# Two-scale attention and two feed-forward layers: four pairs of the first batch in flight instead of two

## The chip, the cores and the metric

The kernel runs on one core of one Trainium2 chip. The metric is the time of one execution on the device in microseconds; the time before is 996.45 us, the median of 3 runs (994.6 to 997.91).

## What is computed

The inputs are q, k and v of 4 batches, 8 heads, 576 tokens and head size 64, and two pairs of weights. Everything is fp32.

```
def sm_attn(qq, kk, vv):  softmax(scale * qq @ kk.T) @ vv, with 1e-9 added to the row sum
q_d, k_d, v_d = means of each 4 tokens of q, k, v          # 144 coarse tokens
out_up    = repeat(sm_attn(q_d, k_d, v_d), 4)              # the coarse scale
out_local = sm_attn(q, k, v) masked to |i - j| < 4         # the local scale
x = (out_up + out_local), heads side by side               # 2304 x 512
x = leaky(x @ w_in1) @ w_out1      # leaky(h) = max(0.01 h, h); w_in 512 x 2048, w_out 2048 x 512
y = x @ w_in2;  out = (y - tanh(y)) @ w_out2
```

## The kernel before

Attention works on pairs of heads: a pair of one batch fills 128 partitions (2 x 64), and there are 16 pairs, four to a batch. The work of a pair is written as 17 steps, 0 to 16, and every engine has its own part of a step (`attention(step, s, i)` in each engine's block; s is the set of buffers, i the count of its use). TensorE turns q and k token groups (steps 0 to 3, line 364), makes the local scores (4, line 371) and the coarse ones (6, line 438), turns the scaled probabilities (11 to 14, lines 390 and 395) and multiplies them with v (15 and 16, lines 403 and 411). ScalarE copies from PSUM and takes the exponentials. VectorE sums q and k over four tokens (3 and 4, lines 815 and 823), adds the mask `band`, takes maxima and sums, subtracts (6, line 833), inverts (8 and 9), and combines both scales into `xT` (15 and 16, line 803). GpSimd sums v over four tokens (step 5, line 985, three instructions), and scales the local (9, line 992) and the coarse probabilities (10, line 997).

The first batch is done before any feed-forward work. `batch0()` writes out its order: at each slot every pair in flight does one step; pair set A starts at slot 0, set B at slot BEHIND = 5, each set handles two pairs one after the other, so there are 39 slots. Within a slot the young steps (below 6) go first. In its last slots set A does the first four steps (HEAD) of the fifth pair. B's buffers lie in `xT` beyond the first batch's columns.

Layer 1 is computed in 8 tiles of 288 tokens. A tile goes through 16 chunks f of the hidden dimension: `hidden1(tile, f)` makes the hidden chunk in `ph1`, `down1(tile, f)` adds its product with w_out into `acc` two chunks later. fp32 is kept by splitting each operand in a high part (ScalarE's copy to fp32r) and a low part (the difference), three matmuls in the place of one. The weights of chunks 0 to 7 are split once and kept (`w_hi_a`, `w_lo_a`; `split_kept`, low part by GpSimd, line 1003); those of 8 to 15 stay whole in `w_whole` and are split again in each tile (`split_in`, `split_out`; low parts by GpSimd, lines 1008 and 1013). In the first six tiles, the mixed ones, two pairs of a later batch are threaded between the chunks: slot 2f and 2f + 1 of 34 stand in chunk f, and slot n does step (n + 4) mod 17. Layer 2 has 6 tiles of 384 tokens.

All loads are issued on the SP queue in a written order: q, k, v of A and B, and then the kept weights 0 to 3 between the loads of the next pairs. `load_v` has two 67-row loads for the outer windows of v (lines 291 and 293), since the first and the last window lack 3 rows, which GpSimd zeroes at the start (line 1050). A queue, and every engine, goes in order: what stands behind a waiting instruction waits too.

Of the kernel before, what the change touches and what calls it, by code (L numbers as in the profile page):

```python
# [57 lines left out]
def two_scale_attention_and_feed_forward(nc, q, k, v, w_in1, w_out1, w_in2, w_out2, out):  # L58
# [36 lines left out]
    with ExitStack() as ctx:  # L95
# [11 lines left out]
        w_hi_a = sb("w_hi_a", [P, KEPT, CW], F32R)  # L107
        w_lo_a = sb("w_lo_a", [P, KEPT, CW], F32R)
# [8 lines left out]
        def second_place(name, shape, at):  # L117
            if name not in in_xT:
                return sb(name + "_b", shape, at=at)
            c, size = in_xT[name], math.prod(shape[1:])  # L120
            start = taken[c]
            taken[c] += size
            assert taken[c] <= TOKENS
            place = xT[0:shape[0], c, start:start + size]
            axes = "abc"[:len(shape) - 1]
            lengths = dict(zip(axes, shape[1:]))
            return place.rearrange(f"p ({' '.join(axes)}) -> p {' '.join(axes)}", **lengths) if len(axes) > 1 else place

# [29 lines left out]
        with ExitStack() as first:  # L158
            banks = ps("banks", [P, 2, 512], at=first)
            A = PairBuffers("a", lambda name, shape: sb(name, shape, at=first), banks)  # L160

            band = sb("band", [P, NB, WIN], at=first)
            ident = sb("ident", [P, P], at=first)
            w_whole = sb("w_whole", [P, WHOLE, CW], at=first)
# [12 lines left out]
            ph1 = ps("ph1", [P, 2, 512], at=first)  # L177


        scratch = sb("scratch", [P, 10 * T2])  # L180
# [5 lines left out]
        w_hi_b = sb("w_hi_b", [P, CF - KEPT, CW], F32R)  # L186
# [41 lines left out]

        def batch0():
# [12 lines left out]
        def later(slot, tile):  # L242

            return (slot + HEAD) % STEPS, A, 2 * tile + 2 + (slot + HEAD) // STEPS

# [25 lines left out]
        def _(sp):  # L271
# [56 lines left out]
            load_qk(A, 3, 10)  # L328
            load_v(A, 3, 10)
            for j in range(WHOLE - 4, WHOLE):  # L330
                load_whole(j)
            with sp.Fori(1, MIXED) as tile:
                for par in range(2):
                    load_qk(A, 2 * tile + 2 + par, 4 * tile + 8 + 2 * par)
                    load_v(A, 2 * tile + 2 + par, 4 * tile + 8 + 2 * par)
            sp.wait_ge(A.bank_free[0], uses0(PAIRS - 2, 0))
# [23 lines left out]
        def _(pe):  # L360
# [54 lines left out]
            def attention(step, s, i):  # L415
# [41 lines left out]
                elif step == 15:  # L457
                    pe.wait_ge(s.v_loaded, 96 * i + 96)
# [72 lines left out]
            def down2(tile, f):  # L531
# [5 lines left out]
                if f < KEPT:  # L537
                    whi, wlo = w_hi_a[:, f, DM:CW], w_lo_a[:, f, DM:CW]
# [36 lines left out]
            pe.wait_ge(B.bank_free[0], uses0(2, 0))  # L575
            pe.wait_ge(B.bank_free[1], uses1(2, 0))
# [13 lines left out]
        def _(act):  # L590
# [104 lines left out]
            def next_x(tile):  # L695
                if not isinstance(tile, int) or tile <= MIXED:
                    act.wait_ge(A.bank_free[0], uses0(2 * tile + 2, 0))
# [11 lines left out]
            def w2a(f):  # L709
                j = f - 4  # L710
                if 0 <= j < KEPT:
                    act.wait_ge(w2a_loaded[j % STAGE_SLOTS], 32 * (j // STAGE_SLOTS + 1))
                    act.wait_ge(y_done, N1 - CF + j + 1)
                    act.activation(w_hi_a[:, j, :], stage[:, j % STAGE_SLOTS, :], ACT.Copy).then_inc(w2_hi_done, 1)
# [59 lines left out]
            act.wait_ge(A.bank_free[0], uses0(2, 0))  # L774
            act.wait_ge(B.bank_free[0], uses0(2, 0))
# [23 lines left out]
        def _(dve):  # L799
# [99 lines left out]
            def mixed(tile, keep_before, slots=2 * STEPS):  # L899
                def between(slot):  # L900
                    if slot < slots:
                        step, s, i = later(slot, tile)
                        attention(step, s, i, (i + 2) // CD, (i + 2) % CD)
# [5 lines left out]
            def w2a(f):  # L909
                j = f - 4  # L910
                if 0 <= j < KEPT:
                    dve.wait_ge(w2_hi_done, j + 1)
                    dve.tensor_tensor(w_lo_a[:, j, :], stage[:, j % STAGE_SLOTS, :], w_hi_a[:, j, :].bitcast(F32),
                                      ALU.subtract).then_inc(w2a_lo_done, 1)
# [31 lines left out]
            for s in (A, B):  # L946
                dve.memset(s.qd_diag[:, :, :, :], 0.0)
                last = dve.memset(s.kT[:, :], 0.0)
# [3 lines left out]
            for _, step, s, i in batch0():  # L952
                attention(step, s, i, (i + 2) // CD if i == 2 else 0, i % 2 if s is A else 2 + i)
# [22 lines left out]
        def _(pool):  # L976
            def attention(step, s, i):
                if step == 5:

                    pool.wait_ge(s.v_loaded, 96 * i + 96)  # L980
# [68 lines left out]
            for s in (A, B):  # L1049
                pool.memset(s.vw[:, :, :, :], 0.0).then_inc(vw_zeroed, 1)  # L1050
# [63 lines left out]
```

## Time and profile before

| | |
|---|---|
| median of 3 runs | 996.45 us (994.6 to 997.91) |
| profiled execution | 992.21 us |
| its span | 990.4 us |
| TensorE busy | 955.1 us, 96% |
| VectorE, ScalarE, GpSimd busy | 583.2, 554.5, 410.9 us |
| DMA | 41.48 MB, mean 42 GB/s |

Busy times are sums over the instructions of an engine; TensorE's instructions overlap and their ends are modelled. The stages: first batch until 67.8 us, layer 1 with six mixed tiles until about 470, two plain tiles until about 580, layer 2 to the end. Times in rows are from the start of the span. PEclk is the clock granted to TensorE as a share of full speed; nothing is listed for it ahead of the first recorded change, and 1.00 stands there.

### The profile page before, as it was taken

How to read it: one execution, taken by the hardware profiler on the slowest of the kernel's cores; microseconds unless marked ns; L12 is line 12 of the kernel's file. 1: busy time of each engine (PE TensorE's matmuls, PEld its weight loads, DVE VectorE, ACT ScalarE, POOL GpSimd, SP SyncE). 2: the span in 40 equal slices, each digit the busy share in tenths (PEclk: the TensorE clock that was granted, in tenths of full speed). 3: DMA queues.
4: the chain of work that ended last, by engine and by line, in shares of the span. 5: the costliest groups of instructions: out<-in, count | busy, mean ns of one | idle time of the engine just before them, and what ended most of it. 6: DMA issues, size and time to landing. Idle time of an engine off the chain costs nothing.

```text
span 990.4 us, 19687 instructions
## 1 busy us (share of the span) xinstructions
PE 955.1 (96%) x6960; PEld 891.5 (90%) x6960; DVE 583.2 (59%) x1066; ACT 554.5 (56%) x1355; POOL 410.9 (41%) x341
## 2 busy tenths in 40 slices
PE   6788999999999999999999999999999999999998
PEld 5678999999999999999999999889899899898996
DVE  5556653663555546536324867876676676766764
ACT  3445544544645536445354767775575666766654
POOL 3446631823625517327071747633233233233232
PEclk9979999999999999999999999999999999999999
DMA  5762421122012201210200302100000000000000
GB/s 125 163 180 64 129 50 26 25 49 49 23 26 49 49 22 26 49 27 1 65 1 23 117 13 85 43 34 0 1 32 1 32 0 0 32 0 0 32 1 32
DMA packets 87222, 41.48 MB, mean 42 GB/s; under 512 B 59777, under 2 KB 80769, under 8 KB 87169
## 3 DMA queue, kind: packets, MB, share of 16 engines
q1 hardware_dynamic: 87168, 40.78, 15.4%
q8 instruction: 33, 0.54, 0.2%
q14 instruction: 21, 0.16, 0.0%
HBM read 36.04 MB, written 4.72 MB: 41 GB/s over the span
## 4 chain that ended last, share of the span: by engine, by line
PE 76%; POOL 6%; ACT 6%; DVE 5%; issue 3%; DMA 2%; SPq 2%; ACTq 0%; POOLq 0%; DVEq 0%
PE ph L473 11%; PE ph L475 11%; PE ph L474 11%; PE acc L549 6%; PE acc L550 6%; PE acc L551 6%; PE acc L502 6%; PE acc L503 5%; PE acc L504 5%; PE banks L371 2%; PE banks L403 2%; DVE g_lo L871 2%; POOL pl L992 2%; PE banks L390 2%; POOL g_lo L1038 1%
## 5 line engine op out<-in xcount | busy, mean ns | idle before, releaser
L1038 POOL TENSOR_TENSOR g_lo<-scratch,g_hi 128x384 fp32r<-128x384 f32 x96 | 125.6, 1309 | 257.7 <-ACT g_hi L663 257.7
L886 DVE TENSOR_TENSOR g<-g,ph 128x288 f32<-128x288 f32 x128 | 57.9, 453 | 187.7 <-ACT g L683 186.8
L1008 POOL TENSOR_TENSOR in_lo<-w_whole,in_hi 128x512 fp32r<-128x512 f32 x64 | 84.0, 1312 | 160.8 <-ACT in_hi L647 159.4
L473 PE MATMUL ph<-x_hi,w_hi_a 128*128 128x288 f32 (+1 forms) x448 | 144.5, 322 | 1.9 <-DVE x_lo L866 1.9
L475 PE MATMUL ph<-x_hi,w_lo_a 128*128 128x288 f32 (+1 forms) x448 | 140.4, 313 | 0.0
L474 PE MATMUL ph<-x_lo,w_hi_a 128*128 128x288 f32 (+1 forms) x448 | 140.3, 313 | 0.0
L683 ACT ACTIVATE g<-ph 128x288 f32<-128x288 f32 x128 | 52.5, 410 | 155.9 <-PE ph L475 154.4
L922 DVE SCALAR_TENSOR_TENSOR scratch<-scratch,ph 128x384 f32<-128x384 f32 x96 | 53.2, 554 | 108.4 <-ACT scratch L728 103.8
L1013 POOL TENSOR_TENSOR out_lo<-w_whole,out_hi 128x512 fp32r<-128x512 f32 x64 | 86.5, 1351 | 56.2 <-ACT out_hi L651 55.6
L727 ACT ACTIVATE scratch<-ph 128x384 f32<-128x384 f32 x96 | 46.8, 488 | 108.4 <-PE ph L475 106.8
L871 DVE TENSOR_TENSOR g_lo<-g,g_hi 128x288 fp32r<-128x288 f32 x128 | 90.5, 707 | 2.7 <-ACT g_hi L663 2.7
L473 PEld LDWEIGHTS ph<-x_hi,w_hi_a 128*128 128x128 f32 x448 | 84.8, 189 | 5.2 <-issue 3.0
L474 PEld LDWEIGHTS ph<-x_lo,w_hi_a 128*128 128x128 f32 x448 | 84.8, 189 | 1.4
L475 PEld LDWEIGHTS ph<-x_hi,w_lo_a 128*128 128x128 f32 x448 | 84.8, 189 | 0.0
L502 PE MATMUL acc<-g_hi,out_hi 128*128 128x288 f32 x256 | 79.1, 309 | 2.5 <-DVE g_lo L871 2.5
L502 PE MATMUL acc<-g_hi,w_hi_a 128*128 128x288 f32 x256 | 78.4, 306 | 2.6 <-DVE g_lo L871 2.6
L473 PE MATMUL ph<-x_hi,in_hi 128*128 128x288 f32 x256 | 78.8, 308 | 0.0
L504 PE MATMUL acc<-g_hi,out_lo 128*128 128x288 f32 x256 | 75.6, 295 | 0.0
L503 PE MATMUL acc<-g_lo,w_hi_a 128*128 128x288 f32 x256 | 75.6, 295 | 0.0
L474 PE MATMUL ph<-x_lo,in_hi 128*128 128x288 f32 x256 | 75.6, 295 | 0.0
L503 PE MATMUL acc<-g_lo,out_hi 128*128 128x288 f32 x256 | 75.5, 295 | 0.0
L504 PE MATMUL acc<-g_hi,w_lo_a 128*128 128x288 f32 x256 | 75.4, 295 | 0.0
(162 smaller groups left out, 2689.9 us busy)
## 6 DMA issues: line engine op xcount, KB each, us to landing
out_dram<-o_stage SPq DMA_DIRECT2D x18, 256.0 KB, 2.0
w_whole<-in_moe_w_in_dram SPq DMA_DIRECT2D x16, 256.0 KB, 4.2
w_whole<-in_moe_w_out_dram SPq DMA_DIRECT2D x16, 256.0 KB, 4.3
qn<-in_q_dram SPq DMA_DIRECT2D x28, 144.0 KB
kn<-in_k_dram SPq DMA_DIRECT2D x28, 144.0 KB
v4n<-in_v_dram SPq DMA_DIRECT2D x28, 144.0 KB
vw<-in_v_dram SPq DMA_DIRECT2D x28, 122.5 KB
scratch<-in_moe_w_in_dram SPq DMA_DIRECT2D x8, 256.0 KB, 2.7
```

Source lines behind the costliest of these rows:

```text
L473: pe.matmul(bank, whi, x_hi[:, c, 0:width], start=(c == 0), stop=False)
L474: pe.matmul(bank, whi, x_lo[:, c, 0:width], start=False, stop=False)
L475: last = pe.matmul(bank, wlo, x_hi[:, c, 0:width], start=False, stop=(c == CD - 1))
L502: pe.matmul(acc[:, c, 0:T1], whi, g1_hi[:, f % 3, :], start=(f == 0), stop=False)
L503: pe.matmul(acc[:, c, 0:T1], whi, g1_lo[:, f % 3, :], start=False, stop=False)
L504: last = pe.matmul(acc[:, c, 0:T1], wlo, g1_hi[:, f % 3, :], start=False, stop=(f == CF - 1))
L549: pe.matmul(acc[:, j, 0:DM], hi, whi, start=(f == 0), stop=False)
L550: pe.matmul(acc[:, j, 0:DM], hi, wlo, start=False, stop=False)
L871: dve.tensor_tensor(g1_lo[:, f % 3, :], g1[:, f % 2, :], g1_hi[:, f % 3, :].bitcast(F32), ALU.subtract).then_inc(g_lo_done, 1)
L1008: pool.tensor_tensor(in_lo[:, f % 2, :], w_whole[:, f - KEPT, 0:DM], in_hi[:, f % 2, :].bitcast(F32), ALU.subtract).then_inc(in_lo_done, 1)
L1013: pool.tensor_tensor(out_lo[:, f % 2, :], w_whole[:, f - KEPT, DM:CW], out_hi[:, f % 2, :].bitcast(F32), ALU.subtract).then_inc(out_lo_don ...
L1038: pool.tensor_tensor(g2_lo[:, f % 3, :], g2[:, f % 2, :], g2_hi[:, f % 3, :].bitcast(F32), ALU.subtract).then_inc(g_lo_done, 1)
```

## The change

Four sets of buffers, A, B, C and D4, each take one pair of the first batch, four slots apart (BEHIND = 4), so the stage has 29 slots and not 39. C and D4 lie where the kept weights from 2 on (`w_hi_a1`, `w_lo_a1`) and part of `w_whole` are put later; their PSUM banks are half of `acc` and `ph1`. In them q and the turned probabilities share a place. `load_whole(0)` therefore waits until C and D4 are done. The kept chunks 0 and 1 are split at slots 23 and 26, not 20 and 25. The loads are issued in another order. Each 67-row load becomes one of 64 and one of 3 rows, so a pair has eight loads of v. GpSimd sums v at step 11, behind both scalings, and not at step 5; this holds for every later pair too. Zeroing is cut to what is read as zero. In the mixed tiles nothing else changes but A's count of pairs (one less).

```
-BEHIND = 5
+BEHIND = 4
-KEPT_SLOTS = (20, 25)
+KEPT_SLOTS = (23, 26)
...
+            with ExitStack() as third:
+                C = PairBuffers("c", third_place("c", third), acc[:, 2:4, :])
+                D4 = PairBuffers("d", third_place("d", third), ph1)
+            w_hi_a1 = sb("w_hi_a1", [P, KEPT - EARLY, CW], F32R)
+            w_lo_a1 = sb("w_lo_a1", [P, KEPT - EARLY, CW], F32R)
+            w_whole = sb("w_whole", [P, WHOLE, CW], at=first)
...
-            for slot in range(2 * STEPS + BEHIND):
-                places = [(at, s) for at, s, last in ((slot, A, 2 * STEPS + HEAD), (slot - BEHIND, B, 2 * STEPS))
-                          if 0 <= at < last]
+            for slot in range(STEPS + 3 * BEHIND):
+                places = [(slot - BEHIND * c, s) for c, s in enumerate(FIRST)
+                          if 0 <= slot - BEHIND * c < (STEPS + HEAD if s is A else STEPS)]
...
-                wait_from(sp, vw_zeroed, 2)
+                wait_from(sp, vw_zeroed, 1 + FIRST.index(s))
...
-                first_win = vh[bass.ds(head, 2), 0:WIN - PAD, :].rearrange("h s d -> s h d")
-                sp.dma_start(s.vw[PAD:WIN, 0, :, :], first_win).then_inc(s.v_loaded, 16)
-                last_win = vh[bass.ds(head, 2), S - QB - PAD:S, :].rearrange("h s d -> s h d")
-                sp.dma_start(s.vw[0:WIN - PAD, NB - 1, :, :], last_win).then_inc(s.v_loaded, 16)
+                for n, row0, token0 in ((0, PAD, 0), (NB - 1, 0, S - QB - PAD)):
+                    for at, rows in ((0, QB), (QB, PAD)):
+                        part = vh[bass.ds(head, 2), token0 + at:token0 + at + rows, :].rearrange("h s d -> s h d")
+                        sp.dma_start(s.vw[row0 + at:row0 + at + rows, n, :, :], part).then_inc(s.v_loaded, 16)
...
             def load_whole(j):
+                if j == 0:
+                    sp.wait_ge(C.bank_free[0], uses0(1, 0))
+                    sp.wait_ge(D4.bank_free[0], uses0(1, 0))
...
-            for load in (load_qk, load_v):
-                load(A, 0, 0)
-                load(B, 0, 4)
+            load_qk(A, 0, 0)
+            load_qk(B, 0, 2)
+            load_v(A, 0, 0)
+            load_qk(C, 0, 4)
+            load_v(B, 0, 2)
+            load_qk(D4, 0, 6)
+            load_v(C, 0, 4)
+            load_v(D4, 0, 6)
             load_kept(0)
-            load_qk(A, 1, 2)
             load_kept(1)
-            load_qk(B, 1, 6)
+            load_qk(A, 1, 8)
             load_kept(2)
-            load_v(A, 1, 2)
             load_kept(3)
-            load_v(B, 1, 6)
-            load_qk(A, 2, 8)
+            load_v(A, 1, 8)
             load_kept(4)
             load_kept(5)
-            load_v(A, 2, 8)
             for j in range(WHOLE - 4):
                 load_whole(j)
...
-                if step == 5:
-                    pool.wait_ge(s.v_loaded, 96 * i + 96)
+                if step == 11:
+                    pool.wait_ge(s.v_loaded, 128 * i + 128)
...
-            for s in (A, B):
-                pool.memset(s.vw[:, :, :, :], 0.0).then_inc(vw_zeroed, 1)
+            for s in FIRST:
+                pool.memset(s.vw[:, 0:NB:NB - 1, :, :], 0.0).then_inc(vw_zeroed, 1)
```

TensorE in the first batch, before, from the coarse scores of the second pair (set B, whose buffers read `xT`) to the fifth set of q turns: the old pair's turned probabilities and values have at most one other pair between them.

```order
L438 MATMUL acc<-xT 96x144 x3
L390 MATMUL banks<-ident,pl 70x128 x5
L395 MATMUL banks<-ident,pd 72x96 x6
L403 MATMUL banks<-pT,vw 64x64 x2
L411 MATMUL banks<-kT,vd 64x144 x4
L403 MATMUL banks<-pT,vw 64x64 x16
L390 MATMUL acc<-ident,xT 70x128 x4
```

The same place after the change (`turned_c`, `turned_d` and `ph` belong to the third and fourth pair; the lines are 32 higher).

```order
L470 MATMUL acc<-xT 96x144 x3
L396 MATMUL acc<-ident,turned_c 128x72 x4
L422 MATMUL banks<-ident,pl 70x128 x4
L403 MATMUL acc<-kT_c,qT_c 128x70
L403 MATMUL acc<-kT_c,qT_c 64x70 x17
L396 MATMUL ph<-ident,turned_d 128x72 x4
L422 MATMUL banks<-ident,pl 70x128 x4
L396 MATMUL ph<-ident,turned_d 128x72 x4
L422 MATMUL banks<-ident,pl 70x128
L427 MATMUL banks<-ident,pd 72x96 x3
```

Turns and scores of the third and fourth pair now stand between the steps 11 to 13 of the first.

GpSimd in the second half of a mixed tile (the first tile's copy of it), before: `vd` is the sum of v, `in_lo` and `out_lo` are the weights' low parts, `pl` and `pd` the scalings.

```order
L1013 TENSOR_TENSOR out_lo<-w_whole,out_hi 128x512
L985 TENSOR_TENSOR vd<-v4n 72x2x2x64
L985 TENSOR_TENSOR vd<-vd,v4n 72x2x2x64 x2
L1008 TENSOR_TENSOR in_lo<-w_whole,in_hi 128x512
L1013 TENSOR_TENSOR out_lo<-w_whole,out_hi 128x512
L1008 TENSOR_TENSOR in_lo<-w_whole,in_hi 128x512
L1013 TENSOR_TENSOR out_lo<-w_whole,out_hi 128x512
L992 TENSOR_TENSOR pl<-pl,rs 128x630
L1008 TENSOR_TENSOR in_lo<-w_whole,in_hi 128x512
L997 TENSOR_TENSOR pd<-pd,rs 96x432
L1013 TENSOR_TENSOR out_lo<-w_whole,out_hi 128x512
L1008 TENSOR_TENSOR in_lo<-w_whole,in_hi 128x512
```

After the change, from the scaling of the local probabilities on.

```order
L1028 TENSOR_TENSOR pl<-pl,rs 128x630
L1044 TENSOR_TENSOR in_lo<-w_whole,in_hi 128x512
L1033 TENSOR_TENSOR pd<-pd,rs 96x432
L1049 TENSOR_TENSOR out_lo<-w_whole,out_hi 128x512
L1021 TENSOR_TENSOR vd<-v4n 72x2x2x64
L1021 TENSOR_TENSOR vd<-vd,v4n 72x2x2x64 x2
L1044 TENSOR_TENSOR in_lo<-w_whole,in_hi 128x512
```

The three instructions of the sum now stand between the low part of w_out's chunk 11 and that of w_in's chunk 14.

## Rows read from the trace of the kernel before

**Rows 1.** The page, busy time, share of the span and instructions of each engine.

```profile
PE 955.1 (96%) x6960; PEld 891.5 (90%) x6960; DVE 583.2 (59%) x1066; ACT 554.5 (56%) x1355; POOL 410.9 (41%) x341
```

**Rows 2.** Windows: PE, PEld, DVE, ACT, POOL busy; PEclk, DMA share, GB/s.

```profile
5.40:67.80 62.40, 47.41 (x484) 41.61 (x485) 35.59 (x64) 27.88 (x83) 22.37 (x22) 0.89 0.61 147
5.40:33.40 28.00, 21.13 (x179) 18.34 (x180) 14.27 (x28) 10.21 (x33) 8.54 (x10) 1.00 0.71 161
...
48.00:50.00 2.00, 1.13 (x18) 0.92 (x14) 1.54 (x4) 0.00 (x0) 1.64 (x2) 0.50 0.67 150
...
210.00:280.00 70.00, 69.16 (x663) 66.46 (x660) 37.80 (x73) 33.75 (x90) 29.64 (x26) 1.00 0.16 38
```

**Rows 3.** Waits of TensorE from 0 to 67.5 us: total, times, longest.

```profile
PE banks L390 <- POOL pl L992: 1.9, 2, 1.0
```

**Rows 4.** Timeline of TensorE in the first batch: start, duration, what, idle before.

```profile
5.38 1.19 PE L364 MATMUL banks<-ident,qn 72*128 72x72 f32 x8 [5.38 <-DMA qn<-in_q_dram]
...
8.96 2.98 PE L371 MATMUL banks<-kT,qT 64*128 64x70 f32 x36 [0.56 <-ACT kT L603]
11.88 1.22 PE L364 MATMUL acc<-ident,qn_b 72*128 72x72 f32 x8
...
23.16 1.06 PE L390 MATMUL banks<-ident,pl 128*70 128x128 f32 x4
...
33.41 0.69 PE L364 MATMUL banks<-ident,qn 72*128 72x72 f32 x4
...
38.73 1.69 PE L371 MATMUL banks<-kT,qT 64*128 64x70 f32 x36 [0.57 <-ACT kT L603]
...
67.81 0.58 PE L473 MATMUL ph<-x_hi,w_hi_a 128*128 128x288 f32 x1 [1.91 <-DVE x_lo L866]
```

**Rows 5.** Timeline of VectorE: last instruction of set A's second pair, and of set B's.

```profile
59.31 0.69 DVE L803 TENSOR_TENSOR xT<-banks,up 128x512 f32<-128x512 f32 x1 [1.15 <-PE banks L403]
...
65.95 0.69 DVE L803 TENSOR_TENSOR xT<-acc,xT 128x512 f32<-128x512 f32 x1 [0.37 <-PE acc L403]
```

**Rows 6.** Timeline of the SP queue: loads of k, and the two 67-row loads of v.

```profile
6.01 1.63 SPq L277 DMA_DIRECT2D kn_b<-in_k_dram  x2
...
9.67 0.33 SPq L291 DMA_DIRECT2D vw<-in_v_dram  x1
10.04 3.21 SPq L293 DMA_DIRECT2D vw<-in_v_dram  x1
```

**Rows 7.** The chain that ended last, within 0 to 90 us: start, duration, what.

```profile
16.70 6.66 DMA xT<-in_v_dram
```

**Rows 8.** Windows: the stretch with only 67-row loads under way.

```profile
18.00:22.00 4.00, 3.08 (x38) 2.79 (x35) 2.33 (x8) 0.03 (x1) 2.65 (x4) 1.00 0.17 39
```

**Rows 9.** Timeline of GpSimd: sum of v, low part of a kept chunk, first later chunk.

```profile
17.29 0.72 POOL L985 TENSOR_TENSOR vd<-v4n 72x256 f32<-72x256 f32 x1 [12.40 <-DMA vw<-in_v_dram]
...
46.07 2.39 POOL L1003 TENSOR_TENSOR w_lo_a<-w_whole,w_hi_a 128x1024 fp32r<-128x1024 f32 x1 [1.21 <-ACT w_hi_a L637]
...
97.28 1.30 POOL L1008 TENSOR_TENSOR in_lo<-w_whole,in_hi 128x512 fp32r<-128x512 f32 x1 [3.39 <-ACT in_hi L647]
```

**Rows 10.** Timeline of VectorE: means of q, and the same subtraction twice.

```profile
35.98 1.51 DVE L815 TENSOR_REDUCE qd_diag<-qT 64x144 f32<-64x576 f32 x2 [2.63 <-ACT qT L597]
...
43.47 0.82 DVE L833 TENSOR_TENSOR pl<-pl,mxl 128x630 f32<-128x630 f32 x1
...
52.20 1.69 DVE L833 TENSOR_TENSOR xT<-xT 128x630 f32<-128x630 f32 x1
```

**Rows 11.** Timeline of GpSimd in the third mixed tile: the sum, and w_in's chunk 14.

```profile
243.72 0.74 POOL L985 TENSOR_TENSOR vd<-v4n 72x256 f32<-72x256 f32 x1
244.54 1.56 POOL L985 TENSOR_TENSOR vd<-vd,v4n 72x256 f32<-72x256 f32 x2
...
258.81 1.29 POOL L1008 TENSOR_TENSOR in_lo<-w_whole,in_hi 128x512 fp32r<-128x512 f32 x1
```

**Rows 12.** Timeline of TensorE: the first matmul of that tile's hidden chunk 14.

```profile
261.65 0.38 PE L473 MATMUL ph<-x_hi,in_hi 128*128 128x288 f32 x1
```

More of the change, by code:

```diff
@@ L123, in second_place, with shaped @@
             assert taken[c] <= TOKENS
-            place = xT[0:shape[0], c, start:start + size]
+            return shaped(xT[0:shape[0], c, start:start + size], shape)
+        def shaped(place, shape):
             axes = "abc"[:len(shape) - 1]
@@ L127, in second_place, with third_place, place @@
             return place.rearrange(f"p ({' '.join(axes)}) -> p {' '.join(axes)}", **lengths) if len(axes) > 1 else place
+        def third_place(which, at):
+            turned = sb("turned_" + which, [P, 2 * RUN * 2 * D], at=at)
+            in_turned = {"qn": 0, "pT": 0, "kn": RUN * 2 * D}
+            def place(name, shape):
+                if name not in in_turned:
+                    return sb(f"{name}_{which}", shape, at=at)
+                start, size = in_turned[name], math.prod(shape[1:])
+                return shaped(turned[0:shape[0], start:start + size], shape)
+            return place
         class PairBuffers:
@@ L159, in two_scale_attention_and_feed_forward @@
             banks = ps("banks", [P, 2, 512], at=first)
+            ph1 = ps("ph1", [P, 2, 512], at=first)
+            with ExitStack() as third:
[4 more added lines that the diff above has]
+            w_whole = sb("w_whole", [P, WHOLE, CW], at=first)
             A = PairBuffers("a", lambda name, shape: sb(name, shape, at=first), banks)
@@ L176, in two_scale_attention_and_feed_forward @@
             g1_lo = sb("g1_lo", [P, 3, T1], F32R, at=first)
-            ph1 = ps("ph1", [P, 2, 512], at=first)
+        w_hi_b = sb("w_hi_b", [P, CF - KEPT, CW], F32R)
         scratch = sb("scratch", [P, 10 * T2])
@@ L242, in later @@
         def later(slot, tile):
-            return (slot + HEAD) % STEPS, A, 2 * tile + 2 + (slot + HEAD) // STEPS
+            return (slot + HEAD) % STEPS, A, 2 * tile + 1 + (slot + HEAD) // STEPS
         def halves_at(f):
@@ L327, in _ @@
             load_kept(7)
-            load_qk(A, 3, 10)
-            load_v(A, 3, 10)
+            load_qk(A, 2, 10)
+            load_v(A, 2, 10)
             for j in range(WHOLE - 4, WHOLE):
@@ L333, in _ @@
                 for par in range(2):
-                    load_qk(A, 2 * tile + 2 + par, 4 * tile + 8 + 2 * par)
-                    load_v(A, 2 * tile + 2 + par, 4 * tile + 8 + 2 * par)
-            sp.wait_ge(A.bank_free[0], uses0(PAIRS - 2, 0))
+                    load_qk(A, 2 * tile + 1 + par, 4 * tile + 8 + 2 * par)
+                    load_v(A, 2 * tile + 1 + par, 4 * tile + 8 + 2 * par)
+            sp.wait_ge(A.bank_free[0], uses0(PAIRS - 3, 0))
             for f in range(KEPT):
@@ L574, in _ @@
                 attention(step, s, i)
-            pe.wait_ge(B.bank_free[0], uses0(2, 0))
-            pe.wait_ge(B.bank_free[1], uses1(2, 0))
+            for s in (B, C, D4):
+                pe.wait_ge(s.bank_free[0], uses0(1, 0))
+                pe.wait_ge(s.bank_free[1], uses1(1, 0))
             mixed(0, begun=False)
@@ L696, in next_x @@
                 if not isinstance(tile, int) or tile <= MIXED:
-                    act.wait_ge(A.bank_free[0], uses0(2 * tile + 2, 0))
+                    act.wait_ge(A.bank_free[0], uses0(2 * tile + 1, 0))
                 split_x(x1_hi, T1, tile, CF * tile)
@@ L713, in w2a @@
                     act.wait_ge(y_done, N1 - CF + j + 1)
-                    act.activation(w_hi_a[:, j, :], stage[:, j % STAGE_SLOTS, :], ACT.Copy).then_inc(w2_hi_done, 1)
+                    act.activation(w_hi_a(j, slice(0, CW)), stage[:, j % STAGE_SLOTS, :], ACT.Copy)\
+                        .then_inc(w2_hi_done, 1)
             def w2b(f):
@@ L902, in between @@
                         step, s, i = later(slot, tile)
-                        attention(step, s, i, (i + 2) // CD, (i + 2) % CD)
+                        attention(step, s, i, (i + 3) // CD, (i + 3) % CD)
                 layer1(tile, between, nothing, keep_before, lambda: next_x(tile + 1))
@@ L944, in keep_out @@
                 dve.tensor_copy(o_stage[:, DM:2 * DM], acc[:, 1, 0:DM]).then_inc(o_kept_dve, 1)
-            for s in (A, B):
+            for s in FIRST:
                 dve.memset(s.qd_diag[:, :, :, :], 0.0)
-                last = dve.memset(s.kT[:, :], 0.0)
+                dve.memset(s.kT[:, 0:PAD], 0.0)
+                last = dve.memset(s.kT[:, PAD + S:PAD + S + PAD], 0.0)
             last.then_inc(zeros_set, 1)
@@ L952, in _ @@
             for _, step, s, i in batch0():
-                attention(step, s, i, (i + 2) // CD if i == 2 else 0, i % 2 if s is A else 2 + i)
+                attention(step, s, i, i, FIRST.index(s))
             lo_of_x(x1_hi, x1_lo, T1, 0, 0)
@@ L1047, in w2b @@
                         .then_inc(w2b_lo_done, 1)
-            for s in (A, B):
-                pool.memset(s.vw[:, :, :, :], 0.0).then_inc(vw_zeroed, 1)
+            for s in FIRST:
+                pool.memset(s.vw[:, 0:NB:NB - 1, :, :], 0.0).then_inc(vw_zeroed, 1)
             pool.memset(ident[:, :], 0.0).then_inc(ident_set, 1)
```

35 lines of the change are left out of this document (19 added, 16 removed).

## The prediction

> **What bounds the kernel now.** I read the busy shares first: TensorE is busy 96% of the span [rows 1], so only idle or half-clock TensorE time can be won. The windows say where that is. In a loop tile it is busy 69.16 of 70.00 us; in the first batch's stretch, from 5.4 to 67.8 us, only 47.41 of 62.40, and VectorE, the next fullest, 35.59 [rows 2]. The table of waits of that stretch has TensorE waiting 1.9 us for GpSimd's scaling of the local scores [rows 3]; its first work waited for the load of q until 5.38 [rows 4]. The stage is a chain of dependent steps with two pairs to fill it. Its pace, from the timeline [rows 4, 5]: a pair entering at 33.41 with one other in flight ends at 59.31 + 0.69 = 60.0, so 26.6 us for its 17 slots, 1.56 us each; layer 1 begins at 67.81, 1.2 us after the end of the batch's last instruction at 65.95 + 0.69.
>
> **The loads.** Now q and k of a pair cost the SP queue two rows of 1.63 us; the loads of v about 0.4 us each, but the one issued behind a 67-row load takes 3.21 [rows 6]. The chain of waits shows such a load of the second pair taking 6.66 us from issue to landing [rows 7], and while only these are out the 16 DMA engines are 0.17 busy at 39 GB/s [rows 8]. That idleness is what the 64 + 3 split removes. The Trainium skill, DMA: Bandwidth & Descriptors, section "Why a DMA increments its semaphore by 16 and not by 1", says the number of engines is the largest divisor up to 16 of the slowest dimension: one engine for 67 rows, 16 for 64, three for 3. The 0.17 of rows 8 agrees with one or a few engines; no row here shows them singly.
> With eight v loads of 0.4 a pair gives the queue 3.3 + 3.2 = 6.5 us. v of the first pair starts at 7.7 as now; q and k of the fourth are issued by 7.7 + 3.2 + 3.3 + 3.2 + 3.3 = 20.7, and land by 23.4, if landing follows as the first did (issued by 2.6, used at 5.38). After v of the third and fourth (6.4), two weight chunks (some 3.3) and 1.6, the fifth pair's q lands at 34.7. Both must be compared with when TensorE asks.
>
> **When the fourth pair starts.** It enters at slot 12, where the first pair's second group of turned scores stands: 23.16 now [rows 4]. Until then GpSimd's sum of v leaves the path: -1.0 (half of the 1.9 us wait; GpSimd had sat 12.40 us on the load of v, then summed it ahead of the scaling [rows 3, 9]). Added are the third pair's sixteen turns, twice the 1.22 us of eight [rows 4], and its VectorE means, 1.51 us [rows 10], each ahead of the older pairs' work in its queue: +3.9. Start 26.1. The load (23.4) is 2.7 ahead. A wait for the coarse scaling, which also stands behind a sum of v, goes too, but behind this point, and lies in the pace below.
>
> **How long it takes.** Lower bound: the 26.6 us of a pair with one other. Upper bound: VectorE sets the pace while three or four are in flight. Its 35.59 us less 1.1 for the x split is 8.6 us a pair; four slots hold one pair's worth, so 2.15 us a slot, nine slots 19.4. The last eight slots hold two pairs or one; the lone pace, from 5.38 to 11.88 over five slots, is 1.3, so 10.4. Together 29.8. Slot 17 comes at 26.1 + 5 x 2.15 = 36.9, after the fifth pair's q (34.7). The weight chunk's low part, 2.39 us of GpSimd [rows 9], now stands ahead of the fourth pair's sum of v, but that sum is asked for four slots later (5.2 us), so I cost it at nothing; without that cover it is 2.39. The stage ends at 52.7 to 55.9, layer 1 begins 1.2 us later: 53.9 to 57.1. I take the middle, 55.5: **-12.3 us** against 67.8 (13.9 to 10.7).
>
> **Costed at nothing.** The smaller zeroing runs before 5.38, while TensorE waits for its first load. The whole-kept weights now load only after slot 28: four chunks of 512 KB, 2.1 MB, 13 us at the 161 GB/s of the early stretch [rows 2]; the first of them was split at 97.28, 29 us after layer 1 began [rows 9]. The kept chunks before them keep their distance to layer 1.
>
> **The sum of v in the loop.** It moves from step 5 to step 11 in every later pair as well. For the first pair of a tile GpSimd is idle there. For the second it falls between the low part of a w_out chunk and that of the w_in chunk 14 (counted from 0). The timeline of a loop tile: the sum takes 243.72 to 246.10, 2.38 us; the w_in low part starts at 258.81 and ends at 260.10 [rows 11]; TensorE begins the chunk that needs it at 261.65 [rows 12]. The slack is 1.55, the sum is 2.38: TensorE waits 0.83. At the old place GpSimd next waits for ScalarE's high part anyway, so nothing is won there. Six tiles: **+5.0 us**. Bounds: 0, if the slack is longer than its timestamps (GpSimd's spans are rough), and 6 x 2.38 = 14.3, if there is none.
>
> **Sum.** -12.3 + 5.0 = -7.3. The profiled execution took 992.21 us (span 990.4): 984.9. The median shown, 996.45, lies 4.2 above it; I carry the difference over: **989.2 us**. A measurement of this kernel can tell 0.3%, 3 us.
>
> **Rivals.**
> *The slack holds* (no new wait in the tiles). For it: four slots of the chunk order lie between, and the rows are GpSimd's. Then -12.3: 984.2.
> *The 3-row loads or the 64-row ones hold the queue as the 67-row ones did.* Each v again costs 2.9 more (3.21 less 0.33). The fourth pair's q and k land at 29.2, the fifth's q at 46.3 against 36.9, and TensorE's queue is in order: the stage loses 9.4, net +2.1: 998.6. Against: rows 8's idle engines.
> *TensorE at its lower clock in the dense slots.* The same scores take 2.98 us at 8.96 and 1.69 at 38.73 [rows 4], and from 48 to 50 us the granted clock is 0.50, the 1.2 GHz level [rows 2]; the early rows list 1.00 but last as long, so I go by durations. 21.13 us of TensorE until 33.4 [rows 2] served one pair and two thirds: 12.7 us a pair at that level, 3.2 a slot. Nine slots cost 9.2 more than VectorE's pace, net +1.9: 998.4. Against: the rows at 38.73 are at full level after TensorE had worked without a gap, and dense slots have fewer gaps.
> *VectorE held up by GpSimd.* The same subtraction takes 0.82 and 1.69 us, the longer one while GpSimd works [rows 10]. If each of the four sums' twelve instructions (0.74, rows 11) delays one of VectorE's on the path, that is 8.9 of the 12.3: net +1.6, 998.1. The Trainium skill, SBUF — State Buffer, speaks for this in its section "Who interferes with whom": an instruction of VectorE with two inputs in SBUF and one of GpSimd that reads SBUF exclude each other for their whole length. The 1.69 us agree. The sums only change place, though, and they delay VectorE now too.
> *Slower:* in the second pair's place of every tile the sum costs its whole 2.38 us, and VectorE's low part of g behind it is stretched by the 0.87 seen in [rows 10], so TensorE's next w_out product waits as well: 6 x 3.25 = 19.5 against 12.3, net +7.2: 1003.7. It decides from 2.05 us a tile upward. Against: the 1.55 us of slack would have to be none.
>
> **Chances.** Forecast 0.50; slack holds 0.25; loads 0.08; clock 0.07; VectorE 0.05; slower 0.05. The forecast's own range, from the stage's bounds, is 987.6 to 990.8, faster by over 3 us throughout; of the middle three rivals a part ends either side. So faster 0.78, within 0.3% 0.15, slower 0.07. The range takes in the slack rival with the short stage (-13.9, so 982.6, and a little below) and up to the partial rivals: 981.5 to 996.5.
>
> **What would show it.** TensorE's first matmul of layer 1 near 55.5 us, not 67.8. VectorE over 0.8 busy between 26 and 45 us. No SP row over 1 us among the loads of v, and DMA shares over 0.6 until 30 us. GpSimd no longer waiting for v ahead of its first scaling. In each of six tiles a TensorE wait of about 0.8 us on GpSimd's low part of w_in; if absent, the slack rival. Layer 2's stretch unchanged. The forecast is wrong if layer 1 starts after 62 us, or the six tiles take over 9 us more than now.

## The result: slower, and the profile after

| | before | changed |
|---|---|---|
| median | 996.45 us | 1005.02 us (1001.76 to 1007.89, 7 runs) |
| ratio | | 1.0091, 95% interval 1.0076 to 1.0106 |
| profiled execution, span | 992.21, 990.4 us | 1007.89, 1006.1 us |
| layer 1 begins | 67.81 us | 66.91 us |
| third mixed tile's x split to the next | 67.5 us | 71.2 us |

I forecast 989.2 us, 0.7% faster. The kernel became 0.9% slower. The stage of the first batch, where I expected 12.3 us, gave 0.9 in the profiled execution, and the six mixed tiles together cost 15.7 us there and not 5.

The table of waits of TensorE in the changed kernel, whole span (total, times, longest):

```profile
PE banks L396 <- DMA qn<-in_q_dram: 12.2, 2, 6.9
PE acc L534 <- DVE g_lo L906: 9.8, 12, 1.9
PE ph L505 <- POOL in_lo L1044: 4.4, 6, 0.9
PE acc L581 <- POOL g_lo L1074: 2.1, 4, 0.7
PE ph L505 <- DVE x_lo L901: 1.9, 1, 1.9
PE banks L422 <- POOL pl L1028: 1.6, 5, 0.3
```

The first line holds the known 5.3 us at the start and a new wait of 6.9. The waits for `in_lo` are new, one in each of the six mixed tiles. Of the twelve for `g_lo`, four of about 1.4 us are new, one in each of the second to fifth mixed tile; the first and the last have none of them. The wait for GpSimd's local scaling in the first batch falls from 1.9 us [rows 3] to 0.3, and that for the coarse scaling, 2.5 us before, is gone.

**The first batch.** Windows of the changed kernel (PE, PEld, DVE, ACT, POOL busy, PEclk, DMA share, GB/s), then TensorE's timeline at slot 17 and at the start of layer 1:

```profile
5.40:34.70 29.30, 26.62 (x293) 22.97 (x293) 21.53 (x37) 13.88 (x39) 9.57 (x10) 1.00 0.77 151
34.70:41.60 6.90, 0.02 (x1) 0.00 (x0) 6.07 (x12) 1.67 (x7) 3.57 (x5) 0.72 0.96 228
41.60:66.90 25.30, 21.68 (x191) 17.90 (x192) 7.05 (x16) 12.07 (x33) 10.38 (x9) 0.50 0.45 110
```

```profile
25.75 0.47 PE L396 MATMUL ph<-ident,turned_d 72*128 72x72 f32 x4
...
41.63 0.74 PE L396 MATMUL banks<-ident,qn 72*128 72x72 f32 x4 [6.91 <-DMA qn<-in_q_dram]
...
66.91 0.58 PE L505 MATMUL ph<-x_hi,w_hi_a 128*128 128x288 f32 x1 [1.93 <-DVE x_lo L901]
```

The fourth pair enters at 25.75, where I had 26.1. Up to 34.7 TensorE is fuller than before (26.6 of 29.3 us against 21.1 of 28.0 [rows 2]). Then its queue stands for 6.9 us at the first instruction of the fifth pair, with all four earlier pairs' work behind it; the DMA engines are 0.96 busy meanwhile. What follows runs at a granted clock of 0.50, the 1.2 GHz level, to the end of the stage, although TensorE is busy 21.7 of these 25.3 us.

The SP queue says why that q is late (start, duration):

```profile
7.71 0.58 SPq L311 DMA_DIRECT2D v4n<-in_v_dram  x1
...
12.18 1.70 SPq L302 DMA_DIRECT2D turned_c<-in_q_dram  x2
...
17.58 3.36 SPq L321 DMA_DIRECT2D xT<-in_v_dram  x4
...
32.80 1.21 SPq L324 DMA_DIRECT2D w_whole<-in_moe_w_in_dram  x1
...
35.99 1.73 SPq L302 DMA_DIRECT2D qn<-in_q_dram  x2
```

v of a pair costs the queue 4.0 to 5.4 us (the first from 7.71 to 12.18), not 3.2: the four window loads take 2.3 to 3.4 together. Taken one by one, a 64-row load costs 0.61 to 0.71 us and a 3-row load 0.46, whatever the pair; only one 64-row load, the first of the second pair, took 1.67. The fifth q is issued at 35.99, behind two weight chunks, and used 5.6 us later.

**A mixed tile.** GpSimd and VectorE in the second tile of the changed kernel (timelines: start, duration):

```profile
190.60 1.28 POOL L1049 TENSOR_TENSOR out_lo<-w_whole,out_hi 128x512 fp32r<-128x512 f32 x1
191.85 0.73 POOL L1021 TENSOR_TENSOR vd<-v4n 72x256 f32<-72x256 f32 x1
192.66 1.55 POOL L1021 TENSOR_TENSOR vd<-vd,v4n 72x256 f32<-72x256 f32 x2
194.17 1.28 POOL L1044 TENSOR_TENSOR in_lo<-w_whole,in_hi 128x512 fp32r<-128x512 f32 x1
195.40 1.30 POOL L1049 TENSOR_TENSOR out_lo<-w_whole,out_hi 128x512 fp32r<-128x512 f32 x1
196.64 1.30 POOL L1044 TENSOR_TENSOR in_lo<-w_whole,in_hi 128x512 fp32r<-128x512 f32 x1
197.88 1.28 POOL L1049 TENSOR_TENSOR out_lo<-w_whole,out_hi 128x512 fp32r<-128x512 f32 x1
```

```profile
189.20 0.67 DVE L906 TENSOR_TENSOR g_lo<-g,g_hi 128x288 fp32r<-128x288 f32 x1
193.16 0.45 DVE L921 TENSOR_TENSOR g<-g,ph 128x288 f32<-128x288 f32 x1 [3.29 <-ACT g L717]
193.53 5.94 DVE L906 TENSOR_TENSOR g_lo<-g,g_hi 128x288 fp32r<-128x288 f32 x1
```

And TensorE's two waits there:

```profile
195.57 0.40 PE L505 MATMUL ph<-x_hi,in_hi 128*128 128x288 f32 x1 [0.64 <-POOL in_lo L1044]
...
199.62 0.37 PE L534 MATMUL acc<-g_hi,out_hi 128*128 128x288 f32 x1 [1.38 <-DVE g_lo L906]
```

The wait for the low part of w_in is the one I forecast, 0.64 us here. The other is new: VectorE's low part of g, 0.45 us of work, took 5.94. It ended at 199.47, when GpSimd's last instruction of the row, 197.88 + 1.28, had just ended. GpSimd goes from 190.60 to 199.16 with no gap longer than 0.1 us. In the same place before the change the subtraction took 1.18 us, and GpSimd's next instruction began 0.12 us after the end of the one before it:

```profile
192.94 1.18 DVE L871 TENSOR_TENSOR g_lo<-g,g_hi 128x288 fp32r<-128x288 f32 x1
```

```profile
192.51 1.30 POOL L1013 TENSOR_TENSOR out_lo<-w_whole,out_hi 128x512 fp32r<-128x512 f32 x1
193.93 1.34 POOL L1008 TENSOR_TENSOR in_lo<-w_whole,in_hi 128x512 fp32r<-128x512 f32 x1
```

A row without a gap is not all that it takes. Between 185.59 and 190.60 GpSimd has no gap either, and `g_lo` took only 0.67 us at 189.20: it ended 0.36 us after GpSimd's scaling of the coarse probabilities had begun at 189.51. And in the first mixed tile of the same kernel, with the same row of GpSimd instructions, `g_lo` took 0.45 us. There it began 0.02 us ahead of the last addition of the sum, and the addition was stretched; in the second tile it began 0.06 us behind it (VectorE first, then GpSimd's addition in the first and in the second tile):

```profile
124.88 0.45 DVE L906 TENSOR_TENSOR g_lo<-g,g_hi 128x288 fp32r<-128x288 f32 x1
```

```profile
124.90 1.03 POOL L1021 TENSOR_TENSOR vd<-vd,v4n 72x256 f32<-72x256 f32 x1
...
193.47 0.73 POOL L1021 TENSOR_TENSOR vd<-vd,v4n 72x256 f32<-72x256 f32 x1
```

The sixth tile passes like the first (0.45 at 476.64, with the addition listed at 476.63 and stretched to 1.05). In the third to fifth tile `g_lo` began 0.06 to 0.07 us behind the addition and took 5.92 to 5.94; in the kernel of run 2 below it began 0.02 us behind it in the first tile and took 5.97. So less than 0.1 us in the order of the two goes with 5.5 us; no run moves this order alone. Why `g_lo` gets past some boundaries of GpSimd's instructions and not past these four, no run here shows.

### The profile page after: what moved, and what is told of

It reads as the page before. It is cut to its first block, busy times and chain, and to the rows that moved or that the text cites. A ratio compares the mean times of both kernels' runs of the same rounds, so it can differ in the third digit from the quotient of the medians.

```text
span 1006.1 us, 19769 instructions
## 1 busy us (share of the span) xinstructions
PE 964.7 (96%) x6960; PEld 897.4 (89%) x6960; DVE 590.0 (59%) x1074; ACT 553.8 (55%) x1355; POOL 413.4 (41%) x343
## 3 DMA queue, kind: packets, MB, share of 16 engines
q1 hardware_dynamic: 87744, 40.78, 15.6%
## 4 chain that ended last, share of the span: by engine, by line
PE 75%; DVE 7%; ACT 5%; POOL 5%; SPq 3%; issue 2%; DMA 2%; ACTq 0%; DVEq 0%
PE ph L505 12%; PE ph L507 11%; PE ph L506 11%; PE acc L581 6%; PE acc L582 6%; PE acc L583 6%; PE acc L534 6%; PE acc L535 5%; PE acc L536 5%; DVE g_lo L906 4%; PE banks L403 2%; PE banks L435 2%; POOL g_lo L1074 1%; PE banks L422 1%; PE banks L396 1%
## 5 line engine op out<-in xcount | busy, mean ns | idle before, releaser
L1049 POOL TENSOR_TENSOR out_lo<-w_whole,out_hi 128x512 fp32r<-128x512 f32 x64 | 90.0, 1407 | 58.9 <-ACT out_hi L685 58.9
L906 DVE TENSOR_TENSOR g_lo<-g,g_hi 128x288 fp32r<-128x288 f32 x128 | 105.1, 821 | 2.7 <-ACT g_hi L697 2.7
```

The costliest lines, as they stand in the source:

```text
L906: dve.tensor_tensor(g1_lo[:, f % 3, :], g1[:, f % 2, :], g1_hi[:, f % 3, :].bitcast(F32), ALU.subtract).then_inc(g_lo_done, 1)
L1049: pool.tensor_tensor(out_lo[:, f % 2, :], w_whole[:, f - KEPT, DM:CW], out_hi[:, f % 2, :].bitcast(F32), ALU.subtract).then_inc(out_lo_don ...
```

## The experiments

The first batch's code is the same in the changed kernel and in runs 1, 3 and 4 below; layer 1 began at 66.91, 65.49, 62.36 and 62.64 us in them. So single profiles of this stage differ by up to 4.6 us, and I go by ratios where it matters. Ratios are to the kernel before; the intervals are of 95%.

**1. The sum's place, undone in the tiles.**

```
-            def attention(step, s, i):
-                if step == 11:
+            def attention(step, s, i, sum_at=11):
+                if step == sum_at:
...
-                        attention(*later(slot, tile))
+                        attention(*later(slot, tile), 5)
```

> The changed kernel with GpSimd's sum of v back at step 5 in the mixed tiles, still at step 11 in the first batch. Theory one: the loss in the tiles is the sum's place. In the changed kernel VectorE's g_lo took 5.94 us at 193.53 while GpSimd went without a gap, and the six tiles took 15.7 us more than before. Then every tile comes back to 67.5 us, and the time falls by 13 to 16, to about 990; layer 1 still starts at 66.9. Rival: the tiles are longer for another reason (the kept weights' new places, eight loads of v a pair instead of six); then the tiles stay at 70 us and the time within 3 us of the changed kernel's 1005.

Measured: 991.42 us, 0.9955 (0.9938 to 0.9972), 13.6 us less than the changed kernel. The starts of VectorE's x split, one tile apart, in this kernel:

```profile
134.91 1.57 DVE L901 TENSOR_TENSOR x_lo<-xT,x_hi 128x288 fp32r<-128x288 f32 x4 [1.65 <-ACT x_hi L690]
202.64 1.57 DVE L901 TENSOR_TENSOR x_lo<-xT,x_hi 128x288 fp32r<-128x288 f32 x4 [1.78 <-ACT x_hi L690]
```

and in the changed kernel:

```profile
137.50 1.57 DVE L901 TENSOR_TENSOR x_lo<-xT,x_hi 128x288 fp32r<-128x288 f32 x4 [1.65 <-ACT x_hi L690]
207.40 1.56 DVE L901 TENSOR_TENSOR x_lo<-xT,x_hi 128x288 fp32r<-128x288 f32 x4 [1.78 <-ACT x_hi L690]
...
278.60 1.57 DVE L901 TENSOR_TENSOR x_lo<-xT,x_hi 128x288 fp32r<-128x288 f32 x4 [1.78 <-ACT x_hi L690]
351.27 1.56 DVE L901 TENSOR_TENSOR x_lo<-xT,x_hi 128x288 fp32r<-128x288 f32 x4 [2.00 <-ACT x_hi L690]
```

The second tile takes 67.73 us in this kernel (the second to fifth 67.5 to 67.7), against 69.90, 71.20 and 72.67 for the second, third and fourth in the changed one. Before the change the third took 67.55:

```profile
204.51 1.56 DVE L866 TENSOR_TENSOR x_lo<-xT,x_hi 128x288 fp32r<-128x288 f32 x4 [1.78 <-ACT x_hi L656]
...
272.06 1.57 DVE L866 TENSOR_TENSOR x_lo<-xT,x_hi 128x288 fp32r<-128x288 f32 x4 [1.78 <-ACT x_hi L656]
```

The tiles' loss is the sum's place; the kept weights' places and the number of loads have no part in it that shows (the six tiles took 405.9 us, and 405.5 before).

**2. The sum's place alone.** The kernel before with one edit.

```
-                if step == 5:
+                if step == 11:
```

> The kernel before with one edit: GpSimd's sum of v at step 11 instead of 5, everywhere. Theory one: each of the six tiles takes 2.2 us more, and some have a stretch at granted clock 0.5 behind the wait; the time rises by 10 to 16 less what the first batch wins (the sum no longer waits ahead of the scaling, up to 4 us). So 1003 to 1009. Rival (other reasons): the tiles stay at 67.5, and the time is 992 to 997.

Measured: 1007.97 us, 1.0123 (1.0105 to 1.0141). In its trace g_lo takes 5.93 us at 193.91 in the same place, and TensorE waits for it in all six mixed tiles. This one line makes more than the whole loss of the change.

**3. Which pair of the tile.** As run 1, but the first pair of each tile keeps its sum at step 11.

```
-                        attention(*later(slot, tile), 5)
+                        attention(*later(slot, tile), 5 if slot >= 13 else 11)
```

> As the first run, but only the second pair of each tile has its sum at step 5; the first pair keeps it at step 11. Theory one with the place in it: at the first pair's place GpSimd is idle before and after, so its run is not longer than the two scalings and the sum; the tiles take 67.5 us, the time equals the first run's within 2 us. Rival: VectorE is held up wherever the sum stands behind the scalings; then each tile takes about 1 us more than in the first run, 5 to 7 us in all.

Measured: 988.51 us, 0.9928 (0.9912 to 0.9945), 2.9 us under run 1, a little more than I had allowed. Its second to fifth tiles take 67.5 to 67.7 us like run 1's. So the second pair's place makes the loss, as forecast. That this kernel is even faster than run 1 comes from the first batch, whose code is the same in both: layer 1 begins 3.1 us sooner in its profile. The windows from the fifth q to layer 1, run 1 first, then this run, hold the same 192 matmuls:

```profile
40.20:65.50 25.30, 21.69 (x192) 17.89 (x192) 8.22 (x18) 12.09 (x33) 12.17 (x11) 0.50 0.43 110
```

```profile
40.10:62.40 22.30, 18.01 (x192) 15.16 (x192) 7.29 (x17) 12.03 (x33) 11.61 (x11) 0.65 0.50 125
```

In run 1 the clock stays at 0.50; here it is back at 1.00 from about 44.5 to 51.4 us. The 3.0 us are the clock. The first mixed tile gives 1.3 of it back (71.4 against 70.0), which I leave open.

**4. How long GpSimd holds VectorE up.** The changed kernel, and one wait more on GpSimd, only in mixed tiles.

```
+                    if f == 13 and between is not nothing:
+                        pool.wait_ge(g_lo_done, CF * tile + f)
```

> The changed kernel with one wait more: in chunk 13 of a mixed tile GpSimd waits for VectorE's g_lo of chunk 12 before it goes on with its low parts. All its work stays, the sum too. Theory: VectorE's g_lo (5.94 us in the changed kernel) is held for as long as GpSimd's instructions follow each other without a gap, not for one of them. The gap lets it through at once: g_lo takes under 2.5 us there, TensorE's 1.4 us wait for it goes, only the 0.6 to 0.8 us wait for in_lo is left, a tile takes 68.2 to 68.6 instead of 69.9 and the time falls by 8 to 11 from 1005, since with a shorter wait the clock falls less often. Rival: the g_lo is late because the pile of GpSimd work itself is late, and a wait only adds to it; then the tiles take 69.9 or more and the time stays or rises.

Measured: 994.23 us, 0.9985 (0.9966 to 1.0004), 10.8 us less than the changed kernel, with no work taken out. Timelines of GpSimd and of VectorE:

```profile
190.20 1.28 POOL L1044 TENSOR_TENSOR in_lo<-w_whole,in_hi 128x512 fp32r<-128x512 f32 x1
191.88 1.29 POOL L1049 TENSOR_TENSOR out_lo<-w_whole,out_hi 128x512 fp32r<-128x512 f32 x1 [0.40 <-DVE g_lo L906]
```

```profile
189.57 2.23 DVE L906 TENSOR_TENSOR g_lo<-g,g_hi 128x288 fp32r<-128x288 f32 x1
```

g_lo passes in the 0.40 us gap that GpSimd leaves, as soon as in_lo ends at 191.48. TensorE's wait for in_lo stays (4.5 us in six places), that for g_lo falls to the level of before (3.3 us in six places, 4.0 before), and the second to fifth tiles take 68.2 to 68.5 us. The rival is out: it was not the pile of work, but that VectorE was not let through the pile. The six tiles make 9.8 us of the 14.3 between the two profiles' spans; most of the rest is the first batch, whose code is the same. The Trainium skill, SBUF — State Buffer, section "Who interferes with whom", says that a VectorE instruction with two inputs in SBUF contends with a GpSimd instruction that reads SBUF, and that the order of issue decides who blocks. The runs agree on both (0.45 us at 124.88, ahead of the addition; 5.94 at 193.53, behind it), but the time is longer than an instruction: from 193.53 four GpSimd instructions began and ended ahead of it.

**5. The fifth pair's q sooner.** Run 1, with two lines of the load order changed.

```
             load_v(C, 0, 4)
+            load_qk(A, 1, 8)
             load_v(D4, 0, 6)
             load_kept(0)
             load_kept(1)
-            load_qk(A, 1, 8)
```

> As the first run, and the loads of q and k of the fifth pair are issued ahead of v of the fourth and of the first two weight chunks. Theory two: TensorE's 6.91 us wait at 34.7 us for that q, with the clock at 0.50 from 37.7 to 71 behind it, is what ate the stage's gain. Then the wait is under 1 us, the scores and values until at least 45 us run at the full level, and layer 1 starts at 56 to 60 us, not 66.9; the time is 7 to 11 us under the first run's. Rival: the clock falls anyway, since from slot 21 on two pairs or one leave TensorE gaps; then layer 1 starts at about 61 to 63 us, 4 to 6 us won. Second rival: DMA is the bound of the stage, and another load is late in its place (v of the fourth pair): 0 to 3 us won.

Measured: 982.80 us, 0.9870 (0.9853 to 0.9886), 8.6 us under run 1.

```profile
34.75 0.42 PE L396 MATMUL banks<-ident,qn 72*128 72x72 f32 x4
...
46.45 1.07 PE L422 MATMUL ph<-ident,pl_d 128*70 128x128 f32 x4 [0.65 <-POOL pl_d L1028]
...
57.89 0.58 PE L505 MATMUL ph<-x_hi,w_hi_a 128*128 128x288 f32 x1 [1.93 <-DVE x_lo L901]
```

No wait at slot 17, and layer 1 begins at 57.89. Four turns take 0.42 us at 34.75 (full level) and 1.07 for the larger ones at 46.45, which took 0.63 at full level: the clock still falls in the tail with one or two pairs, at about 44.6 us (run 1: 39.1). In run 1 TensorE waited 3.5 us for this q and layer 1 began 7.6 later. In runs 3 and 4, with the same first batch as run 1, it waited 5.5 and 5.9 us and layer 1 began 4.5 and 4.8 later than here: there the clock came back for some 7 us behind the wait. So a wait costs more than its length where the clock stays low behind it, and these profiles show it both ways.

**6. The 67-row loads put back** in run 5's kernel.

```
-                for n, row0, token0 in ((0, PAD, 0), (NB - 1, 0, S - QB - PAD)):
...
+                sp.dma_start(s.vw[PAD:WIN, 0, :, :], first_win).then_inc(s.v_loaded, 16)
...
+                sp.dma_start(s.vw[0:WIN - PAD, NB - 1, :, :], last_win).then_inc(s.v_loaded, 16)
```

> The kernel with the fifth q sooner (982.8), with the 67-row loads again in the place of those of 64 and 3 rows. Theory: in this order of loads a 67-row pair holds the SP queue for 3.5 us, the four loads for 2.4 to 2.7, so 1 us a pair; q of the fourth pair lands some 2 us later, of the fifth 3 to 4 us later, and the pile on one DMA engine delays v; layer 1 starts 3 to 8 us later than 57.9, and the time is 986 to 991. Rival: the DMA engines are the bound, not the queue, and the split wins nothing; then 982 to 984.

Measured: 988.68 us, 0.9932 (0.9910 to 0.9955), 5.9 us over run 5; layer 1 begins at 63.00, and TensorE waits for the fourth pair's q and k (0.92 and 0.42 us). These waits are short against the 5.1 us by which layer 1 is later; behind the first of them, from 30 to 42 us, the granted clock is 0.52, and 1.00 in run 5. That the waits made it fall is my reading; no run separates the two.

**7. The split of loads alone,** in the kernel before; the edit is run 6's, turned round.

> The kernel before with the 67-row loads as 64 and 3 rows, nothing else. GpSimd's 12.4 us wait for v of the first pair, and the 6.66 us load of the second pair's window in the chain of waits, should shrink; TensorE's 2.5 us wait for the coarse scaling goes, and layer 1 starts 2 to 5 us earlier than 67.8; the time is 990.5 to 993.5. Rival: nothing on the chain changes, 995 to 996.

Measured: 990.42 us, 0.9945 (0.9925 to 0.9965). GpSimd's first sum in it:

```profile
14.59 1.25 POOL L985 TENSOR_TENSOR vd<-v4n 72x256 f32<-72x256 f32 x1 [9.69 <-DMA vw<-in_v_dram]
```

v is there 2.7 us sooner [rows 9], TensorE's wait for the coarse scaling falls from 2.5 to 0.43 us, and layer 1 begins at 64.47. With two pairs in flight the split alone wins 5.5 us by its ratio, as much as split, four pairs and the late sum of the first batch together in run 1 (4.5 by its own, with intervals that overlap): in the load order of the changed kernel, the third and fourth pair win nothing that shows.

**8. Pairs three slots apart.** Run 5, with BEHIND = 3 and the kept chunks at slots 21 and 24.

> The kernel with the fifth q sooner, with pairs three slots apart instead of four (26 slots; kept chunks at slots 21 and 24). If the number of slots with few pairs (the tail at clock 0.50) sets the time, layer 1 starts 2 to 4 us earlier, 979 to 981. Rival: loads and VectorE set it (the DMA is 0.95 busy from 30 to 45 us, VectorE 14.64 of 15), then TensorE waits for the fourth pair's q instead and the time is 982 to 985.

Measured: 982.17 us, 0.9864 (0.9836 to 0.9893), like run 5. TensorE waits 1.96 and 2.35 us for q of the third and fourth pair; layer 1 begins at 56.65. The rival holds as far as the loads go. The granted clock is 0.51 from 24 to 34 us, around and behind the second of these waits; what part of the loss that is, the run does not show.

**9. The loads in the order of need.** Run 8, with this order.

```
             load_qk(A, 0, 0)
             load_qk(B, 0, 2)
+            load_qk(C, 0, 4)
             load_v(A, 0, 0)
-            load_qk(C, 0, 4)
+            load_qk(D4, 0, 6)
             load_v(B, 0, 2)
-            load_qk(D4, 0, 6)
-            load_v(C, 0, 4)
             load_qk(A, 1, 8)
+            load_v(C, 0, 4)
             load_v(D4, 0, 6)
```

> Pairs three slots apart, and the loads of q and k ordered by when TensorE asks: of A, B, C, then v of A, q and k of D4, v of B, q and k of the fifth pair, v of C and D4. In the run with pairs three apart TensorE waited 1.96 and 2.35 us for the third and fourth q. Theory (loads set the stage): these waits shrink by 2 to 4 us together and layer 1 starts 1 to 4 us before 56.5; 978 to 981. Rival (VectorE's 8.6 us a pair is reached): layer 1 stays at 56 to 57 and the time at 982.

Measured: 979.22 us, 0.9843 (0.9821 to 0.9864). This beats both kernels, by 17 and 26 us of the medians (against the kernel before, 15.6 by the ratio; one of its five runs took 984.64). Windows of its stage and the start of layer 1:

```profile
5.30:30.00 24.70, 23.41 (x195) 20.75 (x196) 16.21 (x30) 10.55 (x32) 5.30 (x6) 1.00 0.77 166
30.00:52.60 22.60, 18.32 (x291) 15.22 (x289) 16.49 (x35) 15.73 (x48) 18.21 (x17) 1.00 0.75 186
```

```profile
52.65 0.37 PE L505 MATMUL ph<-x_hi,w_hi_a 128*128 128x288 f32 x1 [2.12 <-DVE x_lo L901]
```

The clock is granted in full to the end of the stage, also in the last slots with one or two pairs, and layer 1 begins 4.0 us sooner than in run 8.

**10. The sum's place in the first batch.** Run 5, with the sum at step 5 there too.

```
-            def attention(step, s, i, sum_at=11):
+            def attention(step, s, i, sum_at=5):
```

> The kernel with the fifth q sooner (982.8), with the sum of v back at step 5 in the first batch too. If the sum's later place in the first batch is worth what I forecast (1.0 us ahead of the fourth pair, and the coarse scaling's wait), the time rises by 1 to 4 us, since GpSimd waits for v ahead of the scalings. Rival: with the split loads v lands in time, and the place doesn't matter: within 1 us of 982.8.

Measured: 987.27 us, 0.9917 (0.9894 to 0.9940), 4.5 us over run 5, a little more than the 1 to 4 that I had allowed; TensorE waits 2.9 us for the scaling of the local scores, layer 1 begins at 62.07. In the first batch the later sum is right, in the tiles it is wrong.

## Why the prediction was wrong, step by step

**The start of the fourth pair** (26.1) came out right: 25.75. Its parts (-1.0 and +3.9) were not measured one by one.

**The loads** failed first. "With eight v loads of 0.4 a pair gives the queue 3.3 + 3.2 = 6.5 us": v costs 4.0 to 5.4 us. I gave every load 0.4, but a 64-row load costs the queue 0.61 to 0.71 and a 3-row load 0.46, and there is some 0.05 between two loads. "The fifth pair's q lands at 34.7": it was used at 41.6; 5.6 us of the 6.9 late are the queue (issued at 36.0, and by my sum at 30.4, that is 20.7 + 6.4 + 3.3), 1.3 the longer way behind the weights. I had taken issue to landing from the first load of the kernel, with nothing ahead of it. The spare of 2.2 us against the asking at 36.9 was also too large by 2.2, as the slots went faster. My rival of late loads named the right place and the right queue, at a price of 2.9 us a pair where 0.8 to 2.2 came. Its 9.4 us for the stage are near what the stage lost against my forecast (7.8 by run 1's ratio, 11.4 in the profile), but part of that loss is the low clock behind the wait, which it did not have: that nearness is luck. I gave the rival 0.08.

**The pace** of 2.15 us a slot was too slow for the dense slots: the five from 25.75 to the asking at 34.72 took 1.8 each, with VectorE busy 8.71 of 8.95 us. For the tail it was too fast: in run 5, without the wait, layer 1 begins 23.1 us behind slot 17, and my upper bound had 20.2. So run 5 begins it at 57.89, above both my bounds (53.9 and 57.1), with the clock at 0.50 from about 44.6 on. Run 9's 52.65 lies below both, but it has 26 slots and not 29, and does not test them.

**The clock.** I weighed a low clock in the dense slots. It came behind the wait and in the tail, where I gave it no price; run 9 shows that the tail need not have it. In runs 6 and 8, around late loads, it came in the dense slots too (0.52 from 30 to 42 us, 0.51 from 24 to 34).

**The tiles** failed most. The 0.83 us for in_lo was right (4.4 us in six places). The sum +5.0 left out what GpSimd's work without a gap does to VectorE: 5.94 us for 0.45 of work, 1.4 us of TensorE's time in four of the six tiles, and a fall of the clock behind some of these waits:

```profile
268.00:274.00 6.00, 4.67 (x46) 4.35 (x47) 2.35 (x5) 1.55 (x4) 1.97 (x2) 0.72 0.00 0
...
339.00:346.00 7.00, 5.62 (x51) 5.15 (x50) 3.07 (x5) 1.55 (x4) 2.29 (x2) 0.68 0.02 4
```

These windows of the changed kernel follow the waits in the third and fourth tile, the two that take 71.2 and 72.7 us: 1.7 and 3.1 more than 67.5 and their two waits (0.6 and 1.4) make. Measured for the six: 13.6 us (run 1). My slower rival named the place and the g_lo, and set its point at 2.05 us a tile; 13.6 / 6 is 2.3. Its way there was only half right: it had the sum cost its whole 2.38 us, where the waits for `in_lo` are 0.6 to 0.9, and it stretched `g_lo` by 0.87 us and not by 5.5. I gave it 0.05, since I read the 0.87 us of stretch in [rows 10] as the most that one instruction can cost, where a longer row of them was coming.

**The sum** as it came out, by the ratios: stage -4.5 (run 1 against before, not -12.3), tiles +13.6 (the changed kernel against run 1, not +5.0); together +9.1. The two parts share run 1, so that they add up to the ratio's 9.1 is no test of them. The profile puts them otherwise, -0.9 and +15.7: it is the slowest of the seven runs of the changed kernel.

## What to carry to other kernels

Ask of an instruction moved on GpSimd not only who waits for it, but whether it closes the gap in which VectorE's two-input work gets through: work that fits by its sum may still hold VectorE up for the whole row, and a short wait on GpSimd can give the gap back. When more pairs go in flight, write down for each load when it is asked for and sort the queue by that, with issue times taken from rows of the same kind of load, 64 and 3 rows apart. And a wait of TensorE can cost more than its length, by the low clock behind it.

## What the runs showed of the hardware

A VectorE subtraction with both inputs in SBUF took 5.9 us through four GpSimd instructions that came without a gap, and got through in a gap of 0.40 us. It took 0.45 us where it began 0.02 us ahead of a GpSimd addition, and 5.94 where it began 0.06 us behind it.

Four window loads of 64 and 3 rows cost the SP queue little less than two of 67 rows (2.3 to 3.4 us against 0.33 + 3.21 [rows 6]), and still the split is worth 5.5 us alone.

Identical code of the first batch started layer 1 within 4.6 us in four profiles, and a wait of TensorE for the same load was 3.5 us in one and 6.9 in another. In the changed kernel and run 1 the granted clock is 0.50 from that wait to layer 1, and the way from the fifth q to layer 1 takes 25.3 us in both; in runs 3 and 4 the mean is 0.65, and it takes 22.3 and 22.2. So about 3 us of the spread are the clock, and the rest is when the q came (40.1 to 41.6). Why the clock came back in two of the four, the runs don't show. In run 9 it is 1.00 to the end of the stage.
